# Attention head and local units of a fused kernel: where the scores and values of four pooled pairs stand in PSUM, and which tokens share a partition

## What is computed

```python
B, H, S, D = 4, 8, 576, 64;  factor = 4
q_d, k_d, v_d = means of q, k, v over 4 successive tokens      # 144 pooled tokens
out_up = repeat(softmax(q_d k_d^T / 8) v_d, 4)                  # pooled attention
mask = |i - j| < 4                                              # local attention
out_local = softmax(where(mask, q k^T / 8, -1e9)) v
x = (out_up + out_local) as [B*S, H*D]                          # 2304 tokens x 512
y = ((x @ w_a) * (x @ w_b)) @ w_out                             # 1536 wide
h = y @ w_in;  solu = h * softmax(h);  ln = layernorm(solu) * g_ln
out = ln @ w_out2                                               # 1024 wide inside
```

## Time and profile before

| What | us |
|---|---|
| three executions | 790.18, 790.07, 787.93 |
| median | 790.07 |
| the profiled execution, its own time | 787.55 |
| its span from the first to the last instruction | 785.5 |
| PE busy | 754.0 |
| DVE busy | 559.4 |
| ACT busy | 298.3 |
| POOL busy | 211.7 |

### The profile page before, as it was taken

How to read it: one execution, slowest core, us unless ns; L and a number is a source line. 1 busy time by engine, 2 the same in 40 slices (tenths; PEclk the granted TensorE clock), 3 DMA queues, 4 the chain that set the end, 5 groups by cost and what they waited for, 6 DMA issues and landing times.

```text
span 785.5 us, 12269 instructions
## 1 busy us (share of the span) xinstructions
PE 754.0 (96%) x4440; PEld 695.0 (88%) x4440; DVE 559.4 (71%) x975; ACT 298.3 (38%) x819; POOL 211.7 (27%) x260
## 2 busy tenths in 40 slices
PE   6778999898999999999999999999999999999998
PEld 5667889798999999999999999999988888888886
DVE  4579999979968887778687876122467766666663
ACT  3534647254353525344434424234322212222222
POOL 2458897446513421051001111122100000000000
PEclk9959999999999999999999999999999999999999
DMA  9999966595787586683955433636121011011011
GB/s 190 195 226 217 233 160 221 174 310 172 245 236 232 174 243 189 183 213 98 253 168 186 142 120 111 197 112 215 54 67 53 29 55 52 29 55 51 30 41 41
DMA packets 96652, 117.27 MB, mean 149 GB/s; under 512 B 19921, under 2 KB 59603, under 8 KB 96593
## 3 DMA queue, kind: packets, MB, share of 16 engines
q1 hardware_dynamic: 81872, 106.98, 49.2%
q10 hardware_dynamic: 14721, 9.51, 4.2%
HBM read 95.62 MB, written 20.84 MB: 148 GB/s over the span
## 4 chain that ended last, share of the span: by engine, by line
PE 84%; DVE 4%; DMA 4%; POOL 2%; SPq 2%; issue 2%; ACT 1%; ACTq 0%; DVEq 0%; POOLq 0%
PE psum L851 26%; PE psum L853 26%; PE psum L852 25%; PE psum L963 2%; DMA raw<-in_q 2%; PE psum L807 1%; POOL raw L1689 1%; PE psum L787 1%; DMA vd_scratch<-raw 1%; SPq L431 1%; PE psum L818 1%; DVE tmp L1414 1%; POOL raw L1693 1%; DMA raw<-in_v 1%; DVE tmp L1464 1%
## 5 line engine op out<-in xcount | busy, mean ns | idle before, releaser
L851 PE MATMUL psum<-x_hi,w_hi 128*128 128x384 f32 x576 | 199.0, 345 | 2.3 <-POOL w_lo L1701 2.3
L853 PE MATMUL psum<-x_hi,w_lo 128*128 128x384 f32 x576 | 194.1, 337 | 0.0
L852 PE MATMUL psum<-x_lo,w_hi 128*128 128x384 f32 x576 | 193.9, 337 | 0.0
L851 PEld LDWEIGHTS psum<-x_hi,w_hi 128*128 128x128 f32 x576 | 109.2, 190 | 5.3 <-POOL w_lo L1701 2.6
L852 PEld LDWEIGHTS psum<-x_lo,w_hi 128*128 128x128 f32 x576 | 109.3, 190 | 0.0
L853 PEld LDWEIGHTS psum<-x_hi,w_lo 128*128 128x128 f32 x576 | 109.0, 189 | 0.0
L851 PE MATMUL psum<-ab_hi,wo_hi 128*128 128x384 f32 x288 | 100.3, 348 | 3.9 <-issue 3.9
L1381 DVE TENSOR_TENSOR ab_f<-psum,a_sb 128x384 f32<-128x384 f32 x72 | 39.8, 553 | 88.1 <-PE psum L853 62.2
L853 PE MATMUL psum<-ab_hi,wo_lo 128*128 128x384 f32 x288 | 97.3, 338 | 0.0
L852 PE MATMUL psum<-ab_lo,wo_hi 128*128 128x384 f32 x288 | 97.0, 337 | 0.0
L1689 POOL TENSOR_TENSOR raw<-raw 96x256 f32<-96x256 f32 x60 | 57.3, 981 | 119.7 <-DMA raw<-in_q 53.1
(11 more groups left out here) (147 smaller groups left out, 1416.0 us busy)
## 6 DMA issues: line engine op xcount, KB each, us to landing
wo_hi<-wo_hi_scratch SPq DMA_DIRECT2D x53, 256.0 KB, 2.8
wo_lo<-wo_lo_scratch SPq DMA_DIRECT2D x53, 256.0 KB, 3.1
k_u<-in_k SPq DMA_DIRECT2D x11, 576.0 KB
v_u<-in_v SPq DMA_DIRECT2D x11, 576.0 KB
k_u<-in_k SPq DMA_DIRECT2D x17, 288.0 KB
v_u<-in_v SPq DMA_DIRECT2D x17, 288.0 KB
wo_raw<-in_moe_w_out SPq DMA_DIRECT2D x19, 256.0 KB, 4.4
raw<-in_v SPq DMA_DIRECT2D x8, 576.0 KB, 7.6
```

What stands on the lines that cost most here:

```text
L851: mm(dst, wh, xh, start=first, stop=False, skip_group_check=not check)
L852: mm(dst, wh, xl, start=False, stop=False, skip_group_check=not check)
L853: last = mm(dst, wl, xh, start=False, stop=end, skip_group_check=not check)
```

## The change

There are two parts, in the head and in the local units.

**Head.** The scores of pairs 2 and 3 go into banks that pairs 0 and 1 leave once their exponents are made: pair 2 into columns 0 to 143 of banks 0 and 6, pair 3 into columns 256 to 399 of the same two. The turned probabilities use banks 7 and 1 twice, and `head_up` goes into the banks 2 to 5 of the local attention. PE makes the scores of pairs 2 and 3 before it turns anything of pair 0, all four turned copies follow each other on ACT, DVE normalises pairs 2 and 3 before it copies the local values of pair 3, and POOL and SP keep their order.

```diff
-        HP_S, HP_T = [6, 0, 2, 4], [7, 1, 3, 5]
+        HP_S = [(6, 7, 0), (0, 1, 0), (0, 6, 0), (0, 6, 256)]
+        HP_T = [7, 1, 7, 1]
+        HP_U = [2, 3, 4, 5]
+        def hp_scores(c, h):
+            return bank(HP_S[c][h])[0:96, HP_S[c][2]:HP_S[c][2] + SD]
...
             def head_pooled_scores(c):
...
                 if c == 2:
-                    pe.wait_ge(s.h_masked, PPB)
-                    pe.wait_ge(s.h_pT_ready, 2 * PPB)
-                if c == 3:
-                    pe.wait_ge(s.x_local, PPB)
+                    pe.wait_ge(s.hp_exped, 2)
...
             def head_turn_pooled(c):
                 pe.wait_ge(s.hp_normed, c + 1)
+                if c >= 2:
+                    pe.wait_ge(s.hp_pT_ready, c - 1)
...
             head_values(2)
+            head_pooled_scores(2)
+            head_pooled_scores(3)
             head_turn_pooled(0)
             head_turn_p(3)
             head_turn_pooled(1)
+            head_values(3)
             head_up(0)
-            head_values(3)
             head_up(1)
-            head_pooled_scores(2)
-            head_pooled_scores(3)
             head_turn_pooled(2)
...
             head_pooled_exp(1)
+            weight_high(0)
+            head_pooled_exp(2)
+            head_pooled_exp(3)
             head_pT(3)
             head_pooled_pT(0)
             head_pooled_pT(1)
-            weight_high(0)
-            head_pooled_exp(2)
-            head_pooled_exp(3)
+            head_pooled_pT(2)
+            head_pooled_pT(3)
             x_high(0, 0)
```

```diff
-TPP = NT // 128
+ROWS = NT // 128
+TPP, HPP = 6, 2
+UB = NT // TPP
...
-                for t in range(TPP):
-                    last = turn(bank(dst)[:, t * 128:(t + 1) * 128], accT[:, t, (c % 2) * 128:(c % 2 + 1) * 128],
-                                ident[:, :])
+                for t in range(ROWS):
+                    last = turn(bank(XB[c % 2])[:, t * 128:(t + 1) * 128], accT[:, c % 2 * ROWS + t, :], ident[:, :])
...
                     if c == 0 and kind == WA:
-                        pe.wait_ge(s.x_hi_ready, DC * m + i + 1)
-                        pe.wait_ge(s.x_lo_ready, DC * m + i + 1)
+                        parts_ = i + 1 if m == 0 else i // 2 * 2 + 2
+                        pe.wait_ge(s.x_hi_ready, DC * m + parts_)
+                        pe.wait_ge(s.x_lo_ready, DC * m + parts_)
...
-                A(x_hi[:, par, c, :], bank(XB[X_BANK[c]], NT), ACT.Copy).then_inc(s.x_hi_ready, 1)
+                A(x_part(x_hi, par, c), x_turned_part(c), ACT.Copy).then_inc(s.x_hi_ready, 1)
```

## The result

| | us | ratio to the kernel before (95% interval) |
|---|---|---|
| before, median of 7 | 787.93 | |
| changed, median of 7 (781.87 to 787.64) | 784.63 | 0.9951 (0.9934 to 0.9969) |
| changed, a second comparison, median of 11 | 786.28 | 0.9971 (0.9960 to 0.9982) |

The first comparison is the one that the forecast is held against: 784.63 us, 3.9 us faster by the ratio (2.4 to 5.2 by its interval). The second gives 2.3 us (1.4 to 3.2). The two meet between 2.4 and 3.2 us. The forecast was 788.5, with "same" as the likeliest case (0.50) and 785.0 as the lower end of the range: it said no change where there is a gain, and the time lies just outside the range.

What follows compares the result with a forecast made beforehand. Bound: PE's wait at block 2 for POOL's low part, behind raw q's landing. Bytes -1.8, clock +0.8, DVE -0.9, parts +0.35 make -1.55 us, from 790.07 to 788.5; range 785.0 to 791.2 (8 in 10).

Steps and rivals of the forecast that it cites:

- the chain at PE: Head to block 2: raw q's landing, POOL's sums and low part release PE, restarting at 66.5 instead of 68.34.
- a term of 0.9 us: DVE from block 2's gate to 147 us: up to 1.1 us further ahead, shortening PE's waits, worth 0.9 us.
- The head's order: Head: exponents of pairs 2 and 3 made earlier, so PE's head work ends at about 45.9, 6 us earlier.
- 4.7 us hidden: Head's lead of 4.7 us vanishes in PE's wait for POOL's low part of block 2, growing from 2.3 to 5.2.
- The bytes: DMA queue ahead of pooled v's store: 0.393 MB less at 215 GB/s, so everything behind lands 1.8 us sooner.
- The clock: Behind PE's longer wait at block 2: half clock costs more than before, by up to 1.6 us, taken as 0.8.
- The small ones: Mostly free; at tile 0's end the next tile's third group waits for part 3 of x_lo, 0.35 us late.
- The lead stays: Rival: DVE keeps the head's 4.7 us, the waits at 122, 138 and 147 us go, 785.4 us; chance 0.38.
- Narrow loads: Rival: unit (1, 0)'s 32-partition loads run at half rate, v_d and raw q come 3.7 us later, 794.0; chance 0.08.

Runs made afterwards that it cites:

- With the wait taken away and the head as it was: Changed kernel with POOL's low part of block 2 ahead of raw q's sums, DVE's scalar operations replaced or left out, tiles not shifted: 0.9958 of the kernel before.
- the bytes put back: Changed kernel with 384 KB of unused k loaded ahead of the stores of pooled v: 0.9980 of the kernel before.
- the kernel with fewer sums on DVE: Changed kernel with DVE's eight sums of weighted values for tile 1 over 128 of 768 elements, the rest left out: 0.9914 of the kernel before.
- head alone: Kernel before with only the head's new banks and order, units and loads as before: 0.9989 of the kernel before.
- units alone: Changed kernel with the head's old banks and order, the new units and their smaller loads kept: 0.9973 of the kernel before.
- Three kernels with the shift: Changed kernel with a 64-byte tile added: unused 0.9977; used, without DVE's scalar operations 0.9993; also with block 2's low part first 0.9993.

## Why the prediction was wrong

**The bound was put on the wrong engine.** The step that failed is the one that ends the chain at PE: the first part read it through POOL's sums to PE's wait of 2.3 us, and made PE's restart (1.8 us earlier) and PE's clock behind it (0.8 us dearer) the terms of the sum. Two runs speak against it. With the wait taken away and the head as it was, PE is at block 2 2.6 us sooner, DVE's accT where it was, and the time is that of the changed kernel. In the second trace of the kernel before, the wait isn't there, PE restarts 1.6 us sooner, and DVE is where it was. What is passed on to the end is DVE's place, which takes 70 us from gate 2 to accT in nine of the twelve rows; PE is ahead of it and waits somewhere. The row for it stood in the text ("DVE is full all the way"), as a side condition of a term of 0.9 us.

The first half of the chain was right. Raw q, POOL's sums and POOL's run do set the pace up to gate 2, but by holding up DVE, not by PE's wait: the operation on two values ends with the seventh subtraction, and the gate follows 4.5 us behind it. In the changed kernel's second trace DVE came to that operation 1.3 us later than in the first (64.94) and left it 0.5 us later, just as POOL's run began 0.5 us later. So DVE's full row is in part POOL's doing, 5.2 us for two values. That the hold-up, and not DVE's own work, fixes the gate rests on these coincidences and on the bytes put back, which moved run and gate alike; no run took the hold-up away.

**The head's order.** Foreseen: 6 us earlier, the first product at 45.9. Seen: 4.6, at 47.26, and 47.84 in the second trace; the kernel with fewer sums on DVE, whose head is the same, has 43.80, so this place moves by 4 us from execution to execution. The exponents of pair 2 start at 38.92, not 36, since ACT waits 2.2 us for the maxima, which DVE makes only at 37.95, after the local values and the normalising of pairs 0 and 1. DVE, which was to leave the head 4.7 us earlier (its last low part at about 49), left it 2.9 us earlier (50.79 for 53.72). "4.7 us hidden" was half right. PE does lose most of it again, but DVE keeps about 2 us (gate 2 at 74.41 for 76.22, accT 2.1 us earlier, with the head alone). In time the head's part is 0.9 us, with an interval from 0 to 1.8 and 0.7 for an unchanged kernel, so that it is worth anything at all rests on one trace.

**The bytes.** 1.8 us foreseen, with bounds of 1.4 to 1.9; v_d's load was issued 2.65 us sooner (34.58 for 37.23), and the sums of q began 3.0 us sooner (53.27 for 56.30). The term was too small by some 1 us. The bytes were counted right, the rate was not: 0.393 MB put back cost 2.65 us, which is 148 GB/s, and not the 215 of 20 to 28 us. (The rows put back go to 64 partitions in one piece each, so it isn't quite the rate of the rows taken away.) A mean over all that is in the queues isn't the rate of the rows that are taken away.

**The clock.** +0.8 us, where the two traces that the forecast compares have the other sign: PE's lead grows from 2.9 to 4.2 us behind block 2. After the changed kernel's wait of 1.6 us the clock stayed full, while the sum had half a clock there for longer than before. Such a stretch comes and goes by the execution: one of two traces of the kernel before has it at 70 us, and none of the three runs with the smallest edits (head alone, units alone, bytes back) has one there, even after PE's 3.4 us of idleness with the head alone. The kernel with fewer sums has one from 65.2 to 68.6 us, behind a wait of 3.7 us. And DVE's place at accT doesn't show these stretches: from gate 2 on it is 70.0 us in the changed kernel, with one at 89.4, and 69.9 with the head alone, which has none there.

**DVE.** The step's own number was good: a lead of 1.8 + 1.1 = 2.9 us at the gate of block 2, and it was 2.91 (2.4 in the second trace). What it was made of was wrong. It isn't that DVE now meets its blocked stretch while it waits for PE; it is held for 5.21 us as before, with POOL's run and all ahead of it moved. That 1.8 and 1.1 make the 2.9 seen is luck: PE's restart alone came 2.9 us earlier, and no 1.1 was added to it. And this 2.9 was the whole term, not 0.9 on top of 1.8: without the clock's 0.8 the sum is -2.35, which agrees with the second comparison (2.3) by the same luck, and which the first exceeds.

**The small ones.** The third group at the turn of the tile shows as a wait of 0.24 us for x_lo at 150.12; 0.35 was foreseen. The narrower loads of later units stay under cover: 246 GB/s for 278 in 160 to 180 us, and PE didn't wait there.

**The rivals.** "The lead stays" came nearest in time, 785.4 for 784.63, by luck, since it is not what happened: the waits at 119, 135 and 144 us are all there, and the lead at 100 us is 2.4 us, not 4.7. "Narrow loads" fell: the raw rows landed sooner, not later. The window of 20 to 28 us moved 221 GB/s with the loads of 32 partitions in it, for 215 before; that is as the Trainium skill has it (SBUF — State Buffer, "Door 1: The DMA port swizzle"), which gives 32 and 64 partitions nearly the same rate. In 160 to 180 us, where loads went from 128 to 64 partitions among others, the rate fell from 278 to 246 GB/s at a DMA share of 0.82 for 0.84. The same section of the Trainium skill has 328 and 196 for such loads alone; the direction agrees, and how much of the fall is theirs no run here shows.

**The anchor.** The absolute time was built on a median of 790.07 from three executions. Medians of 7 to 34 executions since then lie between 787.93 and 788.82, so 1.3 to 2.1 us of the distance between 788.5 and 784.63 are the anchor's, and not the change's. The rest, 1.8 to 2.6 us, lies in the terms above.

**What stays open.** Why the first comparison gives 0.9951 and the second 0.9971; their intervals overlap. How the gain divides between head and units. What moves the head's end by 4 us between executions. What brings the clock down behind the stall of 2.15 us at 185 us in some traces (some 1.5 us each time) and not in others: each trace that has this stretch has one at 144 to 148 us too, but two traces have only the earlier one. And why DVE's accT and the time differ in size in some rows of the table: the head alone is 2.1 us ahead at accT and 0.9 us in time, its trace being that of the shortest of its twelve executions (785.06).

## What to carry to other kernels

Before a wait of PE is called the bound, ask of the engine that works without a gap beside it where it would be if the wait were gone, and compare its own instructions, the k-th gate with the k-th gate, between two traces. Then look at how long its instructions take: an engine without a gap may be held up by a third one, and two values in 5.2 us say so. A second trace of the same kernel is worth as much as an experiment: what differs between the two (here the wait at block 2 and a stretch at half clock) can't carry a sum. And an edit that adds a tile needs a control that adds only the tile.

## What the runs showed of the hardware

- **Sixty-four bytes.** With all tiles behind a small one 64 bytes higher, four of six kinds of matmuls of 128x512 took longer at the median: w_hi with lnT_hi 397 instead of 390 ns, win_hi with y_hi 394 instead of 390, these weights with the low parts 393 and 392. With the low part of the weights it was 389 and 388. In total it is 1.4 us in 155 us. Three kernels with the shift have this drift, and the one with the same edits and no shift doesn't.
- **Who is held up.** In the changed kernel DVE's operation was held for 5.2 us while POOL ran eight subtractions of 0.69 us without a pause, over seven of them and not for one. It hit a TENSOR_SCALAR of two values and a product of two tiles alike, and no reduction. The Trainium skill (SBUF — State Buffer, "SBUF: two separate sides") has an exclusive lock of the port pair that both share, against DVE's operations with two SBUF inputs too, and this case agrees on who is held; by it the holder keeps the lock for one instruction, and here VectorE was held over about seven.
- **The clock row.** The page of the changed kernel's trace shows a full clock everywhere, and the matmuls still stand at half clock from the head to 55 us:

```profile
PEclk9999999999999999999999999999999999999999
```

```profile
47.26 0.66 PE L872 MATMUL psum<-x_hi,w_hi 128*128 128x384 f32 x1
47.72 0.52 PE L873 MATMUL psum<-x_lo,w_hi 128*128 128x384 f32 x1
48.04 0.52 PE L874 MATMUL psum<-x_hi,w_lo 128*128 128x384 f32 x1
```

  Starts 0.32 us apart are half clock (0.17 at the full one). The trace's record of the clock begins at 55.3 us, with the full clock, and its first change is at 89.4 us; the row shows that first value for the time ahead of it as well. The row is to be checked against the distance of matmuls, at the beginning above all.
